# A fused attention and mixture-of-experts kernel: products with the values in pairs of groups, between scores and transposes

## What is computed

```
scores = scale * np.matmul(q, k.transpose(0, 1, 3, 2))
mask = (rel >= 0) & (rel < window)            # rel = query - key, window = 64
scores = np.where(mask, scores, -1000000000.0)
scores = scores - np.max(scores, axis=-1, keepdims=True)
attn = np.exp(scores)
attn = attn / (np.sum(attn, axis=-1, keepdims=True) + 1e-09)
return np.matmul(attn, v).astype(np.float32)
...
x = _moe_ref(x=x, **moe_kwargs)
return _moe2_ref(x=x, **moe2_kwargs)
```

## Time and profile before

| | us |
|---|---|
| median of 3 runs | 1085.48 |
| lowest, highest | 1083.56, 1085.76 |
| the profiled execution, its time | 1084.6 |
| its span in the trace | 1082.8 |
| TensorE busy in the span | 1067.5 (99%) |
| attention, first to last mask matmul | 5.7 to 95.6 |

### The profile page before, as it was taken

One profiled execution on the slowest core, in us unless ns is written; L12 is line 12 of the kernel. 1 busy time (PEld: TensorE's weight loads), 2 busy tenths in 40 slices (PEclk: granted clock), 3 DMA queues, 4 the chain that ended last, 5 costly groups with the idle time before them and its releaser, 6 DMA issues.

```text
span 1082.8 us, 20088 instructions
## 1 busy us (share of the span) xinstructions
PE 1067.5 (99%) x6053; PEld 933.3 (86%) x6054; DVE 573.6 (53%) x1212; ACT 322.6 (30%) x710; POOL 395.2 (37%) x367
## 2 busy tenths in 40 slices
PE   8999999999999999999999999999999999999997
PEld 7878999999999999999988888888888888888885
DVE  6777335344353452453447675565555556556553
ACT  7997113242332432432452112030303020110222
POOL 4557991220220220220085516070706143240486
PEclk9999999999999999999999999999999999999999
DMA  7876534411311311211084626162615344331576
GB/s 213 270 237 221 168 95 176 136 59 22 126 59 30 116 58 29 97 59 30 11 247 157 171 69 184 39 204 48 193 47 161 83 118 126 85 96 48 157 238 235
DMA packets 199347, 133.18 MB, mean 123 GB/s; under 512 B 128720, under 2 KB 160864, under 8 KB 199296
## 3 DMA queue, kind: packets, MB, share of 16 engines
q1 hardware_dynamic: 177440, 75.14, 25.7%
q10 hardware_dynamic: 16032, 38.47, 10.8%
q0 software_dynamic: 5824, 18.95, 5.1%
HBM read 85.87 MB, written 42.73 MB: 119 GB/s over the span
## 4 chain that ended last, share of the span: by engine, by line
PE 92%; POOL 2%; DMA 1%; ACT 1%; issue 1%; another core or an unknown queue 1%; DVE 1%; POOLq 0%; DVEq 0%; ACTq 0%; SPq 0%
PE bank L819 27%; PE bank L978 20%; PE bank L999 19%; PE bank L851 14%; PE bank L1012 3%; PE bank L765 3%; PE bank L792 2%; PE bank L775 1%; PE bank L759 1%; DMA token_rows_b<-expert_rows,slots_u 1%; ACT p_sb L1146 1%; PE bank L895 1%; POOL token_rows_a L703 0%; DMA mask_sb<-in_c_mask 0%
## 5 line engine op out<-in xcount | busy, mean ns | idle before, releaser
L819 PE MATMUL bank<-x_parts,mlp_weights 128*128 128x384 f32 x1704 | 310.7, 337 | 0.0
L819 PEld LDWEIGHTS bank<-x_parts,mlp_weights 128*128 128x128 f32 x1704 | 298.2, 188 | 6.7
L978 PE MATMUL bank<-expert_parts,xT_high 128*128 (+1 forms) x688 | 216.5, 396 | 0.0
L999 PE MATMUL bank<-expert_parts,hT_high 128*128 (+1 forms) x688 | 212.1, 390 | 1.4 <-DVE hT_low L1708 1.4
L685 POOL TENSOR_TENSOR expert_parts<-raw_expert_a,expert_parts 128x512 fp32r<-128x512 f32 x64 | 81.5, 1307 | 234.5 <-ACT expert_parts L1293 232.2
L851 PE MATMUL bank<-mlp_weights,hidden_parts 128*128 128x512 f32 x648 | 162.1, 394 | 0.0
L999 PEld LDWEIGHTS bank<-expert_parts,hT_high 128*128 128x128 f32 x688 | 129.0, 188 | 28.7 <-issue 2.0
L978 PEld LDWEIGHTS bank<-expert_parts,xT_high 128*128 128x128 f32 x688 | 125.7, 188 | 24.4 <-issue 0.4
L851 PEld LDWEIGHTS bank<-mlp_weights,hidden_parts 128*128 128x128 f32 x648 | 120.1, 188 | 23.4 <-issue 1.0
L978 PE MATMUL bank<-expert_parts,xT_low 128*128 (+1 forms) x344 | 134.3, 391 | 0.0
L999 PE MATMUL bank<-expert_parts,hT_low 128*128 (+1 forms) x344 | 134.1, 390 | 0.0
(11 more groups left out here) (207 smaller groups left out, 1245.5 us busy)
## 6 DMA issues: line engine op xcount, KB each, us to landing
raw_expert_a<-in_w ACTq DMA_DIRECT2D x32, 512.0 KB
raw_expert_b<-in_w ACTq DMA_DIRECT2D x32, 512.0 KB, 4.1
x_row<-routed_rows SPq DMA_DIRECT2D x172, 64.0 KB
expert_rows<-y_row SPq DMA_DIRECT2D x43, 256.0 KB
expert_rows<-zeros SPq DMA_DIRECT2D x4, 2304.0 KB, 11.5
v_sb<-in_v SPq DMA_DIRECT2D x32, 256.0 KB, 3.5
q_sb<-in_qT SPq DMA_DIRECT2D x16, 288.0 KB, 3.7
k_sb<-in_kT SPq DMA_DIRECT2D x16, 288.0 KB, 4.0
```

The lines of the kernel that those rows point to most:

```text
L819: last = nc.tensor.matmul(bank[:, 0:CHUNK], w_sb[:, i, wp, at:at + P], xp[:, par, part, k, :], start=n == 0, stop=n == 3 * KB - 1)
L978: last = nc.tensor.matmul(ps[half][:, 0:512], (xTh, xTl)[xp][:, buf, k, :], ew_sb[:, bass.ds(slot, 1), wp, k * F2 + half * 512:k * F2 + ha ...
L999: last = nc.tensor.matmul(y_bank(t)[:, 0:D], (hTh, hTl)[hp][:, f, :], ew_sb[:, bass.ds(slot, 1), 2 + wp, f * D:(f + 1) * D].rearrange("p a ...
```

## The change

TensorE issues value products in odd steps only, for two groups, G-5 and G-4, and between the scores and the transposes. DVE issues its copies out in even steps only, also two, of G-6 and G-5. One copy out is left over after the last step and is added there. In round 0 TensorE's first pair comes in u = 5 and DVE's first in round 1. No instruction other than these moves, no amount of work changes, and ScalarE's, GpSimd's and SP's orders stay.

```diff
@@
         TO_T, TO_PV = 3, 4
+        assert U % 2 == 0
@@
                     pe_qk(pe, G, m, u)
+                    if u % 2 == 1 and (not first or u > TO_PV):
+                        for back in (TO_PV + 1, TO_PV):
+                            pe_pv(pe, G - back, m if u >= back else m - 1, (u - back) % U)
                     if not first or u >= TO_T:
                         pe_transpose(pe, G - TO_T, (u - TO_T) % U)
-                    if not first or u >= TO_PV:
-                        pe_pv(pe, G - TO_PV, m if u >= TO_PV else m - 1, (u - TO_PV) % U)
@@
                     dve_max(dve, G, u)
-                    if not first or u >= TO_PV + 1:
-                        back = u - TO_PV - 1
-                        copy_out(dve, G - TO_PV - 1, back % U, m if back >= 0 else m - 1)
+                    if u % 2 == 0 and not first:
+                        for back in (TO_PV + 2, TO_PV + 1):
+                            copy_out(dve, G - back, (u - back) % U, m if u >= back else m - 1)
@@
             last = LOOPS * U - 1
+            copy_out(dve, last - TO_PV - 1, U - 2 - TO_PV, LOOPS - 1)
             dve_sums(dve, last, U - 1)
```

## The result

| | us |
|---|---|
| before, median of 6 runs | 1085.07 (1083.56 to 1085.76) |
| changed, median of 6 runs | 1090.28 (1088.58 to 1091.62) |
| ratio changed to before | 1.0052, 95% interval 1.0041 to 1.0063 |
| profiled execution of the changed kernel | 1090.26, span 1088.4 |
| span of before | 1082.8 |

The change makes the kernel slower by 5.2 us. The forecast was slower, by 6.6 us, 1092.1, and its range held the time.

What follows compares the result with a forecast made beforehand. TensorE was nearly full, tied with ScalarE's chain at new items' masks. Terms +2.19, +1.17, +0.40, +2.52, +0.36 sum to +6.64 us: 1084.6 profiled becomes 1091.2, plus 0.9 for the median, 1092.1; range 1089 to 1095.

Steps and rivals of the forecast that it cites:

- The bound: At a new item's first mask in attention, ScalarE's 2.83 us chain ties with TensorE's 2.68, ScalarE ahead by 0.15.
- Half rounds: Attention, mask u=0 to mask u=3 takes 5.86 us, mask u=3 to next u=0 6.12; a round 11.98.
- The stretches: Attention cut at masks: rounds 1 and 2 +2.19 us, rounds 3 and 4 +1.17, four half rounds from 70.60 +2.52.
- sum of squares: Rounds 3 and 4 hold four on TensorE; each delays the next mask by 0.74 us.
- The table loads: Stretch 62.48 to 70.60, where ScalarE loads its tables and TensorE waits for copies: +0.40 us, bounds 0.1 and 0.45.
- TensorE's clock: Rival: the clock falls in the new waits; one round would double some 10 us of matmul time, about 1101; chance 0.02.
- 1.35 us waits: New wait of TensorE for ScalarE's query copy at each mask of u=3 in attention, 1.35 us.
- The end: After 92.04, the path is ScalarE's last exponentials and GpSimd's last normalising: +0.36 us, bounds 0.1 and 0.86.
- Drains saved, nothing waits: Rival: with the query copy off the path, TensorE's saved 3.7 us comes in full, 1081.8 us; chance 0.05.
- Transfers pace the stage: Rival: loads set attention's pace, so TensorE's order hardly counts, no change at 1085.5 us; chance 0.05.
- DVE's doubled copies: Rival: DVE's paired copies out come late, 0.15 to 0.3 us per pair, 3 to 6 on top, near 1096; chance 0.06.
- The signs: Profile after: masks wait for ScalarE's queries, some 11 us in all; ScalarE idles before pT copies of u=1 and u=3.

Runs made afterwards that it cites:

- Queries first in the kernel before: Kernel before, with ScalarE's scaled query copy moved to the head of its step, ahead of the pT copy and exponentials: 1081.96 us, ratio 0.9982.
- value products ahead of the transposes in every step: Kernel before, with one set of value products per step, no pairs, issued between scores and transposes: 1092.61 us, ratio 1.0074.
- pairs behind the transposes: Changed kernel, with value products still paired in odd steps but issued after the transposes: 1085.18 us, ratio 1.0010.
- thinned transfers: SP's 16 xT stores moved behind attention, with ScalarE's query copy first, in the kernel before (1.0090) and with paired value products behind the transposes (1.0080).
- with pairs behind the transposes: Changed kernel with both edits, paired value products issued after the transposes and ScalarE's query copy at the head of its step: 1081.93 us, ratio 0.9978.
- queries first in the changed kernel: Changed kernel, with ScalarE's scaled query copy moved to the head of its step, ahead of the pT copy and exponentials: 1083.31 us, ratio 0.9991.

## Why the prediction was right, step by step

**The bound.** That ScalarE's chain and TensorE's own work tie at the new item's mask was the reading on which all rested. Queries first in the kernel before brought the plain half rounds down to TensorE's own 5.28 us, from 5.31 to 5.43, so it held. The 0.15 read from one place was the largest of them.

**Half rounds.** Forecast 5.86 and 6.12, measured 5.82 (16.56 to 22.38) and 6.00 (22.38 to 28.38). The step mask to transposes in odd steps was put at 1.87 and is 1.78. The whole difference is the pair of products, which took 0.85 up to the transposes, where 0.93 was summed. The value products ahead of the transposes in every step, from the experiment above, show how it divides:

```profile
24.50 0.57 PE L792 MATMUL bank<-pT_sb,v_sb 128*64 128x64 f32 x12
25.00 0.55 PE L775 MATMUL bank<-ident,p_sb 128*128 128x128 f32 x3
25.39 0.33 PE L759 MATMUL bank<-mask_sb,identb 128*128 128x384 bf16 x1
```

One set takes 0.50 to the transposes, as it does to a mask. Two take 0.85, so the second adds 0.35, where 0.43 was charged. In both orders the mask behind such transposes comes 0.38 to 0.39 later instead of 0.32, which nobody charged. Per pair TensorE needs 1.16 + 1.78 + 0.38 = 3.32 us, against 3.52 before: 0.20 saved, 0.17 forecast. That the way out costs 0.07 is not read from an edge without it, as the 0.10 is, but from the time of 12 weight loads, 0.43.

**The stretches.** Rounds 1 and 2: +1.84, forecast +2.19. Rounds 5 (second half) to 7: +2.22, forecast +2.52. Both forecasts are high, by 0.07 to 0.09 per half round, and the second by 0.12 at full clock (0.17 us of it was lost to the low clock, below). The pair of products, 0.08 less, is most of that. The largest miss is rounds 3 and 4: +0.47, forecast +1.17. Their half rounds were forecast 5.86, 7.02, 5.86, 6.60 and are 5.74, 6.77, 5.75, 6.38. One mis-sized term is the sum of squares. It was taken at 0.74 from the earlier trace rows, where it follows value products. Behind transposes it costs less, as the changed kernel's rows show:

```profile
47.68 0.55 PE L776 MATMUL bank<-ident,p_sb 128*128 128x128 f32 x3
48.07 0.81 PE L875 MATMUL bank<-squares_first,ones 128*128 128x384 f32 x2
48.72 0.33 PE L760 MATMUL bank<-mask_sb,identb 128*128 128x384 bf16 x1
```

From 47.68 to 48.72 is 1.04; without a sum it is 0.38, so the sum adds 0.66. Two in the half round of round 3 make 0.16 of its miss of 0.25, and with the one of round 4 they make 0.24 of the 0.70. The rest is spread over the four half rounds, about 0.12 each, as in the plain rounds.

**The table loads.** Forecast +0.40, with one profile at +0.74 and the other, at full clock, at 8.53 - 8.12 = **+0.41**. The difference is the mechanism of a rival that was given 0.02: TensorE's clock. In the first profile of the changed kernel TensorE waits for a pT copy, and then runs at half clock:

```profile
70.04 0.57 PE L793 MATMUL bank<-pT_sb,v_sb 128*64 128x64 f32 x12 [2.40 <-ACT pT_sb L1157]
```

```profile
70.00:71.00 1.00, 0.96 (x15) 0.92 (x16) 0.79 (x3) 0.85 (x6) 1.00 (x2) 0.81 1.17 382
71.00:72.00 1.00, 1.00 (x6) 0.94 (x6) 0.93 (x3) 0.55 (x2) 1.00 (x2) 0.50 0.42 164
```

The mechanism was named, but in the wrong place and for the wrong price. It came behind the table loads, not in the 1.35 us waits, and costs some 0.5 us (0.33 in this stretch, 0.17 in the next half round, 6.17 instead of 6.00), not a whole round at half speed. The reason that it was set aside, that the clock held while TensorE was busy for 5.49 of 8.12 us, overlooked that the change joins idle times: before, TensorE had two waits of 0.93 and 1.14 us in this stretch; now that value products come only in odd steps, it has one of 2.40. That the longer wait is what lowers the clock is not shown: the clock fell behind waits of 2.40, 2.23 and, with the pairs behind the transposes, 2.0 us, and did not in a second profile with 2.40.

**The end.** Forecast +0.36, measured +0.31. GpSimd's last normalising starts 7.70 us after the last edge (7.79 forecast):

```profile
105.03 0.83 POOL L598 TENSOR_TENSOR p_sb<-p_sb,rs 128x384 f32<-128x384 f32 x1 [0.16 <-DVE rs L1410]
```

**The rivals.** *Drains saved, nothing waits* was wrong for this kernel, but the saving is real, as the thinned transfers showed. *Transfers pace the stage* was wrong here; once ScalarE's wait was gone, late keys took 1.7 to 2.4 us. *DVE's doubled copies* cost one wait of 0.3 us in the changed kernel. **The signs.** The masks of u=3 and u=0 wait for ScalarE's queries, 8.9 us in all, where some 11 were named; the trace counts a wait from the modelled end of the last matmul, so the 1.34 us above stand there as 1.18. ScalarE sits idle before the pT copy by 0.62 us in u=1 and 1.08 in u=3, where 0.8 and 1.2 were named. **One claim on the profile was off:** TensorE's busy time in attention was to fall by 3 to 4 us and falls by 1.8 (72.45 to 70.67 over the four stretches, with half-clock matmuls among them). Matmuls overlap and their ends are modelled in these rows, so busy time is a poor witness for time between starts.

**A better order.** Two kernels beat both: queries first alone, 0.9982, and with pairs behind the transposes, 0.9978. Their intervals overlap almost wholly, so nothing says that the pairs help there. The first gains about half of its 2 us at the table loads.

## What to carry to other kernels

Moving work on the full engine can free it and still lose, if the moved work now stands ahead of something that another engine's in-order queue waits for: measure start to start from the producer to the last consumer on both paths, and compare the margins before counting the saving. Here the paths tied within 0.15 us. The transposes came 0.94 us later, TensorE's own work behind them shrank from 2.68 to 1.54 us, and ScalarE's chain from there to the next item's mask stayed at 2.88, so TensorE waits 1.34 us for it. A tie like that can be broken on the other engine: hoisting one independent instruction ahead of a waiting one in ScalarE's queue gained 2.2 us, and none of the three reorderings tried on TensorE alone gained anything. And where a variant gains less than it should, look at the granted clock as well as at the waits.

## What the runs showed of the hardware

- 64-column products between 128-column ones cost TensorE 0.10 us going in (0.42 against 0.32 behind transposes). One set of twelve takes 0.50 us to the next 128-column matmul, mask or transposes alike; two in a row take 0.85. A mask behind transposes that follow such products comes 0.38 to 0.39 after them, not 0.32.
- After 2.40 us idle the granted clock was 0.50 for about three us in one execution (and fell behind 2.0 and 2.23 us in the profiles of pairs behind the transposes and of queries first in the changed kernel), and stayed 1.00 in another of the same kernel with the same idle time. It cost 0.5 us where TensorE waited anyway and 1.60 where it did not.
- A load of keys of 288 KB had a median of 4.0 us to land in the kernel before and 4.4 to 4.7 in three of the orders with pairs (4.0 in both profiles of the changed kernel, and 4.0 with the stores moved out).
